# Attention by tiles of two heads, on the two row halves of TensorE, instead of head by head

## The reference

```python
def _attn_ref(q, k, v, w1, b1, w2):                # q, k, v: (4, 8, 576, 64), float32
    scores = scale * np.matmul(q, k.transpose(0, 1, 3, 2))
    ...
    h = np.maximum(x @ w1 + b1, 0.0)               # x: 576 x 576, from the distance of two positions
    bias = h @ w2                                  # one bias per head
    scores = scores + bias.transpose(2, 0, 1)[None, :, :, :]
    scores = scores - np.max(scores, axis=-1, keepdims=True)
    attn = np.exp(scores)
    attn = attn / (np.sum(attn, axis=-1, keepdims=True) + 1e-09)
    return np.matmul(attn, v)
```

## Time and profile before

| | us |
|---|---|
| median of 3 runs | 1095.83 |
| lowest, highest | 1095.35, 1095.99 |
| the profiled execution | 1096.08 |
| its span | 1094.1 |
| PE busy | 1043.6 (95%) |
| DVE, ACT, POOL busy | 550.8, 504.0, 303.8 |

### The profile page before, as it was taken

How to read it: one execution, slowest core, us unless ns; L and a number is a source line. 1 busy time by engine, 2 the same in 40 slices (tenths; PEclk the granted TensorE clock), 3 DMA queues, 4 the chain that set the end, 5 groups by cost and what they waited for, 6 DMA issues and landing times.

```text
span 1094.1 us, 18925 instructions
## 1 busy us (share of the span) xinstructions
PE 1043.6 (95%) x6936; PEld 924.9 (85%) x6936; DVE 550.8 (50%) x1314; ACT 504.0 (46%) x1081; POOL 303.8 (28%) x536
## 2 busy tenths in 40 slices
PE   5859999999999999999999999999999999999998
PEld 3448777777777789999999999998999999989897
DVE  7838677776767622222223132774444454444543
ACT  6957666676667633121212132554343343443433
POOL 3028677776767554000000023660000000000000
PEclk9979999999999999999999999999999999999999
DMA  4771251342423033000000011320000000000000
GB/s 128 233 206 45 48 149 34 85 112 51 119 63 81 19 118 108 1 0 0 0 0 0 0 39 59 97 77 30 1 1 29 0 29 0 0 29 0 30 1 29
DMA packets 93156, 56.00 MB, mean 51 GB/s; under 512 B 61344, under 2 KB 78752, under 8 KB 93088
## 3 DMA queue, kind: packets, MB, share of 16 engines
q1 hardware_dynamic: 93088, 55.11, 17.6%
HBM read 39.46 MB, written 15.63 MB: 50 GB/s over the span
## 4 chain that ended last, share of the span: by engine, by line
PE 84%; DVE 9%; issue 2%; SPq 1%; ACT 1%; DMA 1%; POOL 1%; ACTq 0%
PE ps L1007 39%; PE ps L1067 18%; PE ps L1035 7%; PE ps L913 7%; PE ps L933 5%; PE ps L945 5%; DVE s_sb L746 3%; DVE xT L797 2%; DVE k_lo L764 2%; PE ps L898 2%; DMA bias_scratch<-p_t 1%; DVE pt_t L755 1%; PE ps L972 1%; PE ps L993 0%; ACT p_t L541 0%
## 5 line engine op out<-in xcount | busy, mean ns | idle before, releaser
L1007 PE MATMUL ps<-x_hi,w_all 128*128 128x384 f32 x1632 | 437.2, 336 | 0.3 <-issue 0.3
L1007 PEld LDWEIGHTS ps<-x_hi,w_all 128*128 128x128 f32 x1632 | 297.0, 188 | 5.3 <-issue 1.0
L1007 PE MATMUL ps<-x_lo,w_all 128*128 128x384 f32 x816 | 273.3, 335 | 0.0
L1067 PE MATMUL ps<-w_all,g_hi 128*128 128x512 f32 x576 | 179.8, 393 | 0.0
L746 DVE CUSTOM_DVE_ANT_0 s_sb<-ps,bias_h 128x576 f32<-128x576 f32 (+1 forms) x160 | 120.3, 753 | 87.2 <-PE ps L933 70.2
L1007 PEld LDWEIGHTS ps<-x_lo,w_all 128*128 128x128 f32 x816 | 153.2, 188 | 3.9
L502 POOL TENSOR_TENSOR w_all<-raw,w_all 128x256 fp32r<-128x256 f32 x104 | 80.3, 802 | 273.9 <-ACT w_all L622 269.7
L578 ACT ACTIVATE probs<-s_sb,row_min 128x576 f32<-128x576 f32 (+1 forms) x160 | 124.6, 779 | 34.4 <-DVE row_min L746 32.9
L469 POOL TENSOR_SCALAR probs<-probs,row_inv 128x512 f32<-128x512 f32 (+1 forms) x160 | 108.2, 689 | 87.3 <-DVE row_inv L726 87.3
L1067 PEld LDWEIGHTS ps<-w_all,g_hi 128*128 128x128 f32 x576 | 106.3, 188 | 19.2 <-issue 1.2
L945 PE MATMUL ps<-ident,probs 128*128 128x128 f32 (+1 forms) x640 | 93.3, 269 | 26.1 <-DVE k_lo L764 13.4
(11 more groups left out here) (87 smaller groups left out, 1384.6 us busy)
## 6 DMA issues: line engine op xcount, KB each, us to landing
bias_scratch<-p_t SPq DMA_DIRECT2D x36, 296.0 KB, 3.7
bias_h<-bias_scratch SPq DMA_DIRECT2D x32, 288.0 KB, 4.2
raw<-in_moe_w_out SPq DMA_DIRECT2D x22, 256.0 KB, 3.1
raw<-in_moe_w SPq DMA_DIRECT2D x18, 256.0 KB, 3.0
out<-o_sb SPq DMA_DIRECT2D x18, 256.0 KB, 2.1
q_in<-in_q SPq DMA_DIRECT2D x32, 128.0 KB, 2.3
k_in<-in_k SPq DMA_DIRECT2D x32, 128.0 KB, 2.4
v_in<-in_v SPq DMA_DIRECT2D x32, 128.0 KB, 2.3
```

The costliest lines, as they stand in the source:

```text
L1007: last = pe.matmul(ps[:, bank, 0:BLK], w[:, at:at + P], x[:, kt, :], start=(kt == 0 and n == 0), stop=(kt == KT - 1 and n == 2))
L1067: last = pe.matmul(ps[:, O_BANK + t, :], g[:, ft % 4, t * P:(t + 1) * P], w[:, wout_d(ft):wout_d(ft) + DM], start=(opens and i == 0), stop ...
```

## The change

Two heads are now worked on together, by slots w of one tile each (80 of them, and 2 to drain). The scores of head 0 use rows 0 to 63 of PE, those of head 1 rows 64 to 127, with three products hi*hi, hi*lo, lo*hi of depth 64, each as 512 keys and 64 keys, the two heads' products issued in turn. All scores of a slot lie in banks 0 to 2, and there is one set of them. Transposes are of 64 rows each, alternately on the two row halves, into two banks. q and k come from memory two heads side by side and are transposed without a copy by POOL; ACT rounds them (`copy_turned`), DVE takes the remainder (`low_turned`). The products with v are cut into five pieces, one in each slot. The inverse of the sums is taken for each tile (POOL adds 1e-9, DVE inverts, POOL multiplies all 576 keys of each head). SP raises `bias_free` first, loads the second group's q and k, and the first biases of both heads, inside the bias stage, and two of the small first loads are issued by ACT.

```diff
+            for e in range(4):
+                sp.sem_inc(bias_free[e], 16)
...
             for s in range(NSUP):
                 store_bias(s)
-                if s >= 4 and (s - 4) % 8 == 7:
-                    first_bias((s - 4) // 8, s - 3)
-            first_bias(T, NSUP)
-            for t in range(NT):
-                load_bias(0, 1, t)
+                if s in (3, 4):
+                    load((q, k)[s - 3], (q_in, k_in)[s - 3], 1)
+                if s == 6:
+                    sp.wait_ge(staged_zero, 1)
+                    load_v(0)
+                if s > 4 and (s - 4) % 8 == 7:
+                    first_bias(0, (s - 4) // 8, s - 3)
+                if s > 4 and (s - 4) % 8 == 0:
+                    first_bias(1, (s - 4) // 8 - 1, s - 4)
+            first_bias(1, T - 1, NSUP - 4)
+            for h in range(2):
+                first_bias(h, T, NSUP)
...
+            def normalise(u):
+                n, r = rows[u % NT], u % RING
+                pool.wait_ge(p_exp, 2 * u + 2)
+                pool.tensor_scalar(row_den[:, r, :], row_sum[:, r, :], 1e-9, 1.0, ALU.add,
+                                   ALU.mult).then_inc(den_ok, 1)
+                pool.wait_ge(inv_ok, u + 1)
+                for h in range(2):
+                    pr = probs[0:n, r, h * S:(h + 1) * S]
+                    pool.tensor_scalar(pr, pr, row_inv[0:n, r, h:h + 1], 1.0, ALU.mult, ALU.mult).then_inc(p_norm, 1)
...
+            def copy_turned(w):
+
+                act.wait_ge(xs_ps, XS_COUNT[w])
...
+                    act.activation(qk_hi[:, i % 2, :, t * P:t * P + m * HALF].rearrange("p a (r j) -> p r a j", r=m),
+                                   ps[:, XS_BANK:XS_BANK + m, HALF:3 * HALF].rearrange("p r (a j) -> p r a j", a=2),
+                                   ACT.Copy).then_inc(hi_ok, 1)
...
+            def slot(w):
+                i, t = w // NT, w % NT
+                if t == 2 and i >= 1:
+                    output(i - 1, 0)
+                if t == 0 and i >= 2:
+                    output(i - 2, 1)
+                if w < NU:
+                    exponent(w, 0)
+                if tile_of(w) is not None:
+                    copy_upper(tile_of(w))
+                if w < NU:
+                    exponent(w, 1)
+                copy_turned(w)
...
+            def low_turned(j):
+
+                i, t = j // NT, j % NT
+                m = row_halves(t)
+                at = slice(t * P, t * P + m * HALF)
+                dve.wait_ge(hi_ok, j + 1)
+                dve.tensor_tensor(qk_lo[:, i % 2, :, at].rearrange("p a (r j) -> p r a j", r=m),
...
+            def inverse(u):
+
+                r = u % RING
+                dve.wait_ge(den_ok, u + 1)
+                if u >= RING:
+                    dve.wait_ge(p_norm, 2 * (u - RING) + 2)
+                dve.reciprocal(row_inv[:, r, :], row_den[:, r, :]).then_inc(inv_ok, 1)
+
+            def slot(w):
+                if w < NU:
+                    add_bias(w, 0)
+                    add_bias(w, 1)
+                if tile_of(w) is not None and tile_of(w) % NT < T:
+                    copy_lower(tile_of(w))
+                if turn_of(w) is not None:
+                    low_turned(turn_of(w))
+                if w < NU:
+                    inverse(w)
...
+            def scores(u):
+                i, t = u // NT, u % NT
+                if t == 0:
+                    pe.wait_ge(lo_ok, NT * (i + 1))
+                if u == T:
+                    pe.wait_ge(pads_zero, 2)
+                if u:
+                    pe.wait_ge(s_bias, 2 * u)
+
+                score(0, True, 0, u)
+                score(1, False, 0, u)
...
+            def turn_rest(w):
+
+                u, j = tile_of(w), turn_of(w)
+                pe.wait_ge(lo_ok, min(w + NT, NU))
+                if u is not None:
+                    pe.wait_ge(tail_cp, u)
...
+            VALUES = {0: (0, (0, 1)), 1: (0, (2, 3, 4)), 2: (1, (0, 1)), 3: (1, (2, 3)), 4: (1, (4,))}
```

More of the change, by code:

```diff
@@ L504, in low_weights @@
                 last.then_inc(w_ok, 1)
[L506 to L509 removed]
+            for u in range(NU):
+                normalise(u)
             pool.wait_ge(w_ok, 1)
@@ new lines, in turn_in, with first_turn @@
+            def turn_in(to, x_in, par, t):
+                n = row_halves(t)
+                return [pe.transpose(to[:, r, :], x_in[HALVES[r], par, t, :, :].rearrange("p a d -> p (a d)"),
+                                     ident[HALVES[r], HALVES[r]]) for r in range(n)]
+            def first_turn():
+                pe.wait_ge(qk_in[0], 128)
+                for t in range(NT):
+                    at = pair_at(TURN) if t < T else pair_at(TURN + 1)
+                    for a, x_in in enumerate((q_in, k_in)):
+                        c = (t % T * 2 + a) * HALF
+                        ends = turn_in(ps[:, at:at + 2, c:c + HALF], x_in, 0, t)
+                    for end in ends:
+                        end.then_inc(turn_ps, 1)
@@ L969, in step @@
-                if par == 0 and has(m, 2):
-                    bank = open_slot("tail")
-                    for t in range(T):
-                        last = pe.transpose(ps[:, bank, t * P:(t + 1) * P],
-                                            p_tail[:, t, :, :].rearrange("p a d -> p (a d)"), ident[:, :])
-                    last.then_inc(t_ps, 1)
+                for kt in units:
+                    for h in range(2):
+                        last = pe.matmul(ps[h * HALF:(h + 1) * HALF, O_BANK_A, 0:cols.stop - cols.start],
+                                         v_in[:, i % 2, h, kt, :],
+                                         pt_t[:, i % 2, cols] if kt == T else p_t[:, i % 2, h, kt, cols],
+                                         start=(kt == 0), stop=(kt == T))
@@ L976, in _, with slot @@
+                if units[-1] == T:
+                    last.then_inc(o_ps, 1)
+            def slot(w):
+                i, t = w // NT, w % NT
+                if w < NU:
+                    scores(w)
+                if w == 0:
+                    pe.wait_ge(bias_sb, NSUP)
+                if tile_of(w) is not None:
+                    turn_probs(tile_of(w))
+                turn_rest(w)
+                if i >= 1:
+                    values(i - 1, *VALUES[t])
             pe.wait_ge(ident_ok, 1)
@@ L1020, in first_item @@
                 last.then_inc(c_h, 1)
-            for m in STEPS[1:]:
-                step(m)
-                if m == PAIRS:
-                    first_item(0)
+            for w in SLOTS:
+                slot(w)
+            first_item(0)
+            values(GROUPS - 1, 1, range(NT))
             first_item(1)
```

571 lines of the change are left out of this document (236 added, 335 removed).

## The result

| | before | after |
|---|---|---|
| median of 4 runs, same chip | 1095.59 us | 1117.05 us |
| lowest to highest | 1094.01 to 1095.99 | 1116.46 to 1117.78 |
| profiled execution; its span | 1096.08; 1094.1 | 1116.46; 1114.7 |
| mean granted clock | 0.993 | 0.96 |

The ratio is 1.0199, with a 95% interval of 1.0181 to 1.0217: the changed kernel is slower by about 2%. Forecast were 1074 us and a range from 1062 to 1093.

The account below looks back on a forecast made before the run. PE bounded attention before; after the change a chain through ACT and DVE would. 60.5 + 279.8 + 13.4 + 13.4 = 367.1 us to the second expert item, 21.9 us earlier, gave 1074 us, range 1062 to 1093.

Parts of the forecast that it names:

- The chain: ACT and DVE work from one slot's first add to the next: 3.79 us, 279.8 us over 75 slots.
- the last slots: The last five slots, with nothing left to turn: 3.34 us each, four to the last add, 13.4 us.
- POOL's addition: POOL's addition of 1e-9 ahead of the inverse in the last slots, taken as 0.3 us, between 0.1 and 0.67.
- What is hidden: Work covered by ACT's chain in each slot: PE through by 3.0 of 3.79 us, a cover of 0.7 us.
- Rival D: The clock falls with PE 75% busy in gaps under 1 us; over 1200 us should 1.2 GHz last; 3%.
- PE's work: PE's scores, transposes, values and changes of array form: 2.8 us a slot instead of 3.86.
- rival A: PE's row halves don't overlap: 4.3 us a slot, 1124 us, from 1105 to 1140; 8%.
- 64-key products: Score products of 64 columns on PE, taken as 0.065 us each from the 64-column transposes.
- Rival B: PE stays the bound and all of its saving is seen: 2.8 us a slot, 1005 us; 5%.
- C's forms: Rival: copies across two banks, writing runs of 64, cost 0.2 to 0.35 us more a slot; 1089 to 1100; 9%.
- The ends: First add at 60.5 us (57.7 to 62.7); from last add to second expert item 13.4 us (12 to 17).
- The halt: PE's halt for loads between 62 and 79 us; it goes and gives most of the 21.9 us gain.

Follow-up runs that it names:

- experiment 1: The changed kernel with every tile of q and k turned one slot earlier, an extra slot ahead of the first; 1079.55 us.
- experiment 4: experiment 1 with only the hi*hi score products, eight of twelve score products left out of each slot; 1079.03 us.
- experiment 2: The changed kernel with nine unread float32 products on PE ahead of the wait at a group's first scores; 1105.14 us.
- experiment 10: experiment 7 with the wait for the tail copy moved to the last piece of each half's values, which alone reads the tails; 1047.37 us.
- experiment 3: The kernel before, with q and k of the third and fourth head loaded inside the bias stage; 1089.46 us.
- experiment 7: experiment 6 with five unread float32 products on PE in each slot of the first group; 1057.83 us.
- experiment 5: experiment 1 with DVE's remainder behind the next slot's first add, the inverse behind its second, and PE's values ahead of its transposes; 1075.01 us.
- experiment 6: experiment 5 with ACT's copies of finished outputs moved to slots t = 1 and t = 4, behind the block copy; 1063.09 us.
- experiment 9: experiment 7 with each slot's transposes of probabilities issued as eight on one row half, then eight on the other, instead of alternating; 1064.88 us.

## Why the prediction was wrong

**The chain: right.** Eight terms, each within 0.02 us, sum 3.77 for 3.79; the last slots 3.34 as forecast (386.34 to 389.68), with 0.23 us from POOL's addition to the inverse, for which no row of before existed and 0.3 was taken; 279.56 us for 75 slots in experiment 1, for 279.8, where two small differences happen to cancel. Experiment 4 shows that it, not PE, sets this beat.

**The step that failed** is "What is hidden": "The scores of slot w + 1 wait for both adds of slot w, out of PSUM some 1.4 us after the slot begins ... PE is through by 3.0 of 3.79." At every fifth slot they wait for more: `if t == 0: pe.wait_ge(lo_ok, NT * (i + 1))`, a line that stands in the diff. With the last tile turned in the slot ahead, that semaphore comes 3.23 us after the slot's add (162.28 to 165.51), plus the remainder itself. The rule that the section on the chain used, what stands in front of the add, should have been asked of PE too: for each wait in `scores`, what raises it last, and in which slot. The price could have been had from rows of before: the remainder done at 3.40 (3.49 less the inverse), 0.9 of scores with nothing over them, and some 0.4 in which the last product ends (the length of one in the earlier trace rows), 4.7 instead of 3.49. 15 of these are 18 us, so 1092 at full clock, the end of the range. Measured is 5.12 at full clock (experiment 2) and 5.0 to 6.0 in the change.

**The clock: right in kind, priced at the wrong place.** Rival D had 3%, for a clock that falls because of "gaps under 1 us". The gap in the change is 2.43 us, made by the same wait, and the falls cost 12 to 15 us (experiment 2), about a third of the loss. Here D and the missed wait are one event; but experiment 4 shows falls with no gap over 0.93 us too, so D's reason, though not its price, has something for it.

**PE's work: 3.2, not 2.8 a slot.** The overlap of the halves is real (156.70 is a product of head 1, 156.72 one of head 0), so rival A falls; with the rule that the prediction takes from the Trainium skill ("TensorE: Matmul & The Clock Gate", Part 3), that row tiles run concurrently, the trace agrees. The known error is the 64-key products: on one half they start 0.11 us apart (156.50 to 156.61), not 0.065. Three of them explain 0.14 of the 0.23 us by which a slot's scores are longer (1.13 for 0.9); the rest stays open. In four slots of five this is off the path in the change; at a group's start, where nothing covers the scores, it is on it, 15 x 0.23 = 3.5 us of the wait's 23. In experiment 10 both candidates for the path contain them. Rival B, all of PE's saving seen, was never near. C's forms cost what their rows of before said (tail copy 0.16, rounding 0.40).

**The ends.** ACT's first copy starts at 9.44 instead of 13.38, without its wait for `bias_free`, and DMA from 22 to 62 us is at 87% instead of 79%, yet the first add comes at 62.34, 0.4 us earlier, almost the upper bound. The granted clock there is 0.91 where it was 1.00, so PE may share in that; no run separated the two. The halt went, but taking it out of the kernel before gives 5.6 us (experiment 3), not most of 21.9. The clock is at half in the first group (66.9 to 87.4 us), which costs little while ACT's chain binds: in experiment 1 the first two groups are together 1.7 us longer than two others. It costs 5.3 us only where the chain is cut (experiment 7).

**In numbers:** of the 42.3 us, 37.1 are 15 groups of 21.13 instead of 18.65 (some 23 the uncovered wait, nearly all of the rest the clock), 1.8 the first add, 3.4 the end.

## What to carry over

When a change replaces an engine's bound by a chain, list every wait of every engine at every position of the loop, the first and last of a group above all: a wait that is harmless in four slots of five sets the price in the fifth. A producer should be a full slot ahead of its consumer where covering work depends on it; here one slot's distance was worth 37.5 us. And once a bound is removed, look for waits and copies that stand in an engine's order ahead of what they don't serve: moving them gave 27 us more (experiments 5, 6 and 10).

## What the runs showed of the hardware

- The granted clock was 1.00 up to and through a single idle stretch of PE of 2.43 us (163.43 to 165.85), and 0.52 right behind it (165.80 to 169.20), though PE was busy 85% of the group. In other groups the fall came later: PE was idle from 100.89 to 103.31, worked 1.17 us at 1.00 and then 3.41 us at 0.50. So the price falls now on the long slot (5.0 to 6.0), now on the one behind it (3.8 to 5.0). With the stretch filled by unread products the clock stayed at 1.00 (experiment 2); those nine products a group are worth 12 us. A long gap isn't needed: in experiment 4 the clock was at 0.50 from 136.3 to 143.1 us with no gap over 0.93 us since 84 us.
- Products on two row halves overlap: two of 512 columns start 0.02 us apart (156.70 and 156.72). On one half, those of 64 columns in the rounded type start 0.11 us apart (156.50 to 156.61), while float32 transposes of 64 columns on alternate halves start 0.034 apart, a pair in 0.069 (16 in 0.55 us, the second view in experiment 9).
- Products of one row half can start ahead of earlier ones in the program that use the other half (171.72 and 171.83 in experiment 9; in the change 156.70, of head 1, starts ahead of 156.72, of head 0, which stands first in `scores`). The Trainium skill ("TensorE: Matmul & The Clock Gate", Part 3) says that products start and end strictly in the order of the program; these rows don't agree for starts, and no run here tests the ends, which are modelled.
